# Router logits with the gate weights stationary, four token tiles at a time in quarters of the TensorE array

## What is computed

```python
# attention: 4 batches, 8 heads (4 local, 4 strided), 576 tokens each, head size 64
x = attention(q, k, v)                       # (2304 tokens, 512)
logits = x @ w_gate                          # w_gate is (512, 8)
logits = logits - logits.max()               # one maximum over all tokens and experts
P = np.exp(logits)
for _ in range(8):
    P /= P.sum(1, keepdims=True) + 1e-09
    P /= P.sum(0, keepdims=True) + 1e-09
    P *= N / E
for e in range(E):                           # 8 experts, 1024 wide
    out += P[:, e:e + 1] * (np.maximum(x @ w1[e], 0.0) @ w2[e])
return elu(out @ w_in) @ w_out               # 2048 wide
```

## Time and profile before

| What | us |
|---|---|
| median of 3 runs | 2053.81 (2052.08 to 2055.09) |
| the profiled execution | 2048.03 |
| span of its profile | 2046.2 |
| TensorE busy | 2020.0 (99% of the span) |
| VectorE, GpSimd, ScalarE busy | 1436.3, 1164.6, 903.0 |

### The profile page before, as it was taken

One profiled execution on the slowest core, in us unless ns is written; L12 is line 12 of the kernel. 1 busy time (PEld: TensorE's weight loads), 2 busy tenths in 40 slices (PEclk: granted clock), 3 DMA queues, 4 the chain that ended last, 5 costly groups with the idle time before them and its releaser, 6 DMA issues. The chain is left out here.

```text
span 2046.2 us, 29801 instructions
## 1 busy us (share of the span) xinstructions
PE 2020.0 (99%) x10611; PEld 1825.7 (89%) x10611; DVE 1436.3 (70%) x2462; ACT 903.0 (44%) x1659; POOL 1164.6 (57%) x1519
## 2 busy tenths in 40 slices
PE   7999999999999999999999999999999999999999
PEld 6889999999999999998999998999999999998988
DVE  5776877666667676666666778776666666778876
ACT  5763333333333343333333477433333333477775
POOL 3455755555555565555555567676555555657663
PEclk9999999999999999999999999999999999999999
DMA  7622212222221222212212221222122222221221
GB/s 138 132 63 73 73 62 62 73 72 62 66 79 62 62 64 81 63 62 73 73 62 63 72 72 63 93 72 73 62 62 78 67 62 73 73 63 62 93 73 52
DMA packets 159299, 147.69 MB, mean 72 GB/s; under 512 B 64432, under 2 KB 126128, under 8 KB 159152
## 3 DMA queue, kind: packets, MB, share of 16 engines
q1 hardware_dynamic: 159152, 145.79, 24.1%
HBM read 141.05 MB, written 4.72 MB: 71 GB/s over the span
## 5 line engine op out<-in xcount | busy, mean ns | idle before, releaser
L498 POOL TENSOR_TENSOR w_lo<-w_raw,w_hi 128x256 fp32r<-128x256 f32 x480 | 354.9, 770 | 750.5 <-ACT w_hi L847 750.5
L1116 DVE SCALAR_TENSOR_TENSOR acc<-psum,prob_eps,acc 128x512 f32<-128x512 f32 x516 | 387.0, 750 | 275.7 <-PE psum L722 269.1
L720 PE MATMUL psum<-w_hi,h_hi 128*128 128x512 f32 x1440 | 563.2, 391 | 0.6 <-issue 0.6
L722 PE MATMUL psum<-w_hi,h_lo 128*128 128x512 f32 x1440 | 563.3, 391 | 0.0
L721 PE MATMUL psum<-w_lo,h_hi 128*128 128x512 f32 x1440 | 561.3, 390 | 0.0
L661 PE MATMUL psum<-x_hi_a,w_hi 128*128 128x384 f32 x1296 | 438.4, 338 | 4.2 <-DVE c L1083 3.5
L664 PE MATMUL psum<-x_hi_a,w_lo 128*128 128x384 f32 x1296 | 438.3, 338 | 0.0
L663 PE MATMUL psum<-x_lo_a,w_hi 128*128 128x384 f32 x1296 | 437.0, 337 | 0.0
L491 POOL TENSOR_TENSOR w_lo<-s_tmp,w_hi 128x256 fp32r<-128x256 f32 x480 | 357.7, 776 | 0.0
L722 PEld LDWEIGHTS psum<-w_hi,h_lo 128*128 128x128 f32 x1440 | 270.3, 188 | 58.1
L720 PEld LDWEIGHTS psum<-w_hi,h_hi 128*128 128x128 f32 x1440 | 270.3, 188 | 43.9 <-issue 0.9
(11 more groups left out here) (118 smaller groups left out, 2743.0 us busy)
## 6 DMA issues: line engine op xcount, KB each, us to landing
w_raw<-in_moe_w_dram SPq DMA_DIRECT2D x192, 512.0 KB, 3.6
w_raw<-in_moe_w_in_dram SPq DMA_DIRECT2D x24, 512.0 KB, 3.4
w_raw<-in_moe_w_out_dram SPq DMA_DIRECT2D x24, 512.0 KB, 3.7
v_l<-in_v_dram SPq DMA_DIRECT2D x24, 128.0 KB, 3.6
out_dram<-acc SPq DMA_DIRECT2D x2, 1536.0 KB, 6.2
raw_l_q<-in_q_dram SPq DMA_DIRECT2D x8, 288.0 KB, 5.1
raw_l_k<-in_k_dram SPq DMA_DIRECT2D x8, 288.0 KB, 5.8
raw_s_q<-in_q_dram SPq DMA_DIRECT2D x16, 144.0 KB
```

The source lines that it names most:

```text
L498: pool.tensor_tensor(w2_lo[n % 2][piece], w2_raw[piece], w2_hi[n % 2][piece].bitcast(f32), ALU.subtract).then_inc(w2_lo_s, 1)
L720: pe.matmul(dst, h_hi[:, i, kk, js], w2_hi[s][:, i, :], start=(i == 0), stop=False)
L722: mm = pe.matmul(dst, h_lo[:, i, kk, js], w2_hi[s][:, i, :], start=False, stop=(i == 1))
L1116: ins = dve.scalar_tensor_tensor(a, y, 1.0 if bare else gate_of(n, j), a, ALU.mult, ALU.add)
```

## The change

`gate_raw` becomes `gate_pad`: each chunk's 8 gate columns with 24 zero columns beside them, so 32. `logit_round(r)` takes four token tiles at a time (the last round two). For each feature chunk it issues one matmul per tile, all with the same 128x32 block of `gate_pad` as the stationary operand and the tile's 128x128 of `xT` streamed past it; tile j writes partitions 32j to 32j+31 of one 128-column stretch of the `AUX` bank, which sets it to quarter j of the array's columns. The result is the transposed logits. ScalarE copies it to `logits_t` (`logit_copy`), and `select_logits(r)` turns it back with one matmul, `logits_t` stationary and chosen columns of the identity streamed, into the same columns of `AUX` as before. 18 tiles become 5 rounds: at steps (1, 4), (2, 4), (3, 4), with their selections at (1, 5), (2, 5), (3, 5), and two late ones. Three more edits: the gate's load waits for a memset of `gate_pad`, `make_t(0, 2)` waits for two rounds rather than six tiles, and `top_to_row` stands behind `p7(0)`.

```diff
+    QUARTER = P // 4
+    ROUNDS = -(-TT // 4)
...
-        gate_raw = sb("gate_raw", [P, DC, E], f32)
+        gate_pad = sb("gate_pad", [P, DC, QUARTER], f32)
+        logits_t = sb("logits_t", [P, 2, P], f32)
...
+        LOGIT_AT = {(1, 4): 0, (2, 4): 1, (3, 4): 2}
+        SELECT_AT = {(1, 5): 0, (2, 5): 1, (3, 5): 2}
+        LOGIT_LATE = range(len(LOGIT_AT), ROUNDS)
...
-                    sp.dma_start(gate_raw[:, :, :], w_gate.rearrange("(c p) e -> p c e", p=P)).then_inc(gate_in, 16)
+                    sp.wait_ge(gate_zeros, 1)
+                    sp.dma_start(gate_pad[:, :, 0:E], w_gate.rearrange("(c p) e -> p c e", p=P)).then_inc(gate_in, 16)
...
-                        pool.wait_ge(logit_ps, GT)
+                        pool.wait_ge(logit_t, -(-GT // 4))
...
-            def logit(tt, batch):
-                pe.wait_ge(x_done, GROUPS * (batch + 1))
+            def logit_round(r):
+                pe.wait_ge(x_done, GROUPS * -(-(4 * r + round_tiles(r)) * P // S))
+                dst, _ = logit_views(r)
                 for c in range(DC):
-                    mm = pe.matmul(bank(AUX)[:, tt * E:(tt + 1) * E], xT[:, c, tt * P:(tt + 1) * P],
-                                   gate_raw[:, c, :], start=(c == 0), stop=(c == DC - 1))
-                mm.then_inc(logit_ps, 1)
+                    for j in range(round_tiles(r)):
+                        t0 = (4 * r + j) * P
+                        mm = pe.matmul(dst[j * QUARTER:(j + 1) * QUARTER, :], gate_pad[:, c, :], xT[:, c, t0:t0 + P],
+                                       start=(c == 0), stop=(c == DC - 1))
+                mm.then_inc(logit_t, 1)
+
+            def select_logits(r):
+
+                pe.wait_ge(logit_copied, ROUNDS if r in LOGIT_LATE else r + 1)
+                n = round_tiles(r)
+                chosen = ident[0:QUARTER * n, 0:QUARTER * n].rearrange("p (j e) -> p j e", j=n)[:, :, 0:E]
+                pe.matmul(bank(AUX)[:, 4 * r * E:(4 * r + n) * E].rearrange("p (j e) -> p j e", e=E), logit_views(r)[1],
+                          chosen, start=True, stop=True).then_inc(logit_ps, 1)
...
-            for tt in LOGIT_LATE:
-                logit(tt, B - 1)
+            for r in LOGIT_LATE:
+                logit_round(r)
             p2(0)
+            for r in LOGIT_LATE:
+                select_logits(r)
+            p7(0)
             top_to_row()
-            p7(0)
             p4(0)
...
+            def logit_copy(r):
+                act.wait_ge(logit_t, r + 1)
+                if r not in LOGIT_LATE[1:]:
+                    wait(act, logit_ps, r)
+                src, dst = logit_views(r)
+                act.activation(dst, src, ACT.Copy).then_inc(logit_copied, 1)
...
                 if n < U:
                     snap(n)
+                if u == -1:
+                    for r in LOGIT_LATE:
+                        act.wait_ge(logit_t, ROUNDS)
+                        logit_copy(r)
```

More of the change, by code:

```diff
@@ L220, in build @@
         x_done = sem("x_done")
+        gate_zeros = sem("gate_zeros")
+        logit_t = sem("logit_t")
+        logit_copied = sem("logit_copied")
         logit_ps = sem("logit_ps")
@@ L290, in build, with round_tiles, logit_views @@
         W0_S, W0_HI_A, W0_HI_S, W0_LO_A, W0_LO_S = (3, 3), (3, 3), (3, 4), (3, 4), (3, 5)
-        LOGIT_AT = {}
-        tt = 0
-        for b in range(B - 1):
-            g = 5
-            while (tt + 1) * P <= (b + 1) * S:
-                LOGIT_AT[b + 1, g] = tt
-                tt, g = tt + 1, g + 1
-        LOGIT_LATE = range(tt, TT)
+        LOGIT_AT = {(1, 4): 0, (2, 4): 1, (3, 4): 2}
+        SELECT_AT = {(1, 5): 0, (2, 5): 1, (3, 5): 2}
+        LOGIT_LATE = range(len(LOGIT_AT), ROUNDS)
+        def round_tiles(r):
+            return min(4, TT - 4 * r)
+        def logit_views(r):
+            rows = QUARTER * round_tiles(r)
+            late = r - LOGIT_LATE[0] if r in LOGIT_LATE else 0
+            return bank(AUX)[0:rows, (2 + late) * P:(3 + late) * P], logits_t[0:rows, late, :]
         def x_splits(n):
@@ L434, in _ @@
             pool.memset(ones[:, :], 1.0).then_inc(ones_made, 1)
+            pool.memset(gate_pad[:, :, :], 0.0).then_inc(gate_zeros, 1)
             pool.memset(prob_eps[:, 0:TT, E:E + 1], EPS).then_inc(eps_made, 1)
@@ L747, in _ @@
                     fill(*f)
-                if (b, g) == (1, 5):
+                if (b, g) == (1, 4):
                     pe.wait_ge(gate_in, 16)
+                if (b, g) in SELECT_AT:
+                    select_logits(SELECT_AT[b, g])
                 if (b, g) in LOGIT_AT:
-                    logit(LOGIT_AT[b, g], b - 1)
+                    logit_round(LOGIT_AT[b, g])
                 if (b, g) == (B - 1, GROUPS):
@@ L913, in _ @@
                     exps(b, g)
+                if (b, g) in LOGIT_AT:
+                    logit_copy(LOGIT_AT[b, g])
                 if (b, g) in X0_HI:
@@ L1183, in _ @@
                 if u == -1:
-                    dve.wait_ge(logit_ps, TT)
+                    dve.wait_ge(logit_ps, ROUNDS)
                     dve.tensor_copy(logits[:, :, :], bank(AUX)[:, 0:TT * E].rearrange("p (t e) -> p t e", e=E))\
```

## The result

| What | before | after |
|---|---|---|
| median of 12 runs each, us | 2050.28 (2047.89 to 2055.09) | 2054.68 (2052.04 to 2060.70) |
| the profiled execution | 2048.03 | 2053.71 |
| span of its profile | 2046.2 | 2051.9 |
| from the first to the last copy or sum of a down projection | 1870.66 | 1876.24 |

The ratio, with its 95% interval in brackets, is 1.0024 [1.0015, 1.0032]: the changed kernel is slower by a quarter of a per cent, where I had forecast 0.22% faster.

A forecast was written before the change was run, and what follows sets the result against it. TensorE was taken as the bound from 180 us, so an earlier start would reach the end in full. Gains of 2.4 us (attention) and 2.2 us (behind it) sum to 4.6: 2053.81 to 2049.2 us, range 2045.8 to 2052.5.

The forecast's parts named there:

- the slower one: Router rounds: quarters run one after another and the clock falls in them; 2056.7 us, or 2065 at worst; chance 0.05.
- The attention's 2.4 us: Attention: three tiles removed from (3, 6) to (3, 8) gain 2.5 us, less 0.1 us for the selection's wait.
- The growing wait at (1, 9): Attention, batch 1: TensorE reaches strided v earlier, so its 0.44 us wait becomes 1 to 2 us; gain 0.
- The selection at (3, 5): Attention, batch 3: waits for ScalarE's copy behind the exponential of (3, 4), ends at about 131.1; cost 0.1 us.
- R: Length of the late rounds behind the attention, 48 records; taken as 3.0 us, bounds 1.75 and 5.2.
- Rival 1: Router rounds: four quarters run at once, R = 1.75; gain 5.8 us, 2048.0 us; chance 0.2.
- Rival 2: Router rounds: quarters run one after another, R = 5.2; gain 2.0 us, 2051.8 us; chance 0.2.
- `p4(0)` at R + 5.5: Behind the attention: p4(0) starts 5.5 us plus R after the late rounds start, held by VectorE's queue; before, 10.86 us.
- The idle 0.7 us: Behind the attention: TensorE stands idle 0.7 us before top_to_row, until VectorE's copy and maximum end at R + 3.4.
- The 0.2 us for changes of shape: Behind the attention: three changes between array shapes, 0.1 us each or less, cost 0.2 us in all.
- The cover of `p6(1)`: Behind the attention: GpSimd's splits end at R + 8.2, p6(1) comes at R + 9.2, leaving 1 us.
- Rival 3: Behind the attention: the clock falls anyway, costing 1.5 us; gain 3.1 us, 2050.7 us; chance 0.12.

The follow-up runs named there:

- the new tiles last: Changed kernel with gate_pad and logits_t declared behind all other tiles and 128 unused bytes in gate_raw's place; 2043.45 us, ratio 0.9970.
- the serial run: Kernel with the new tiles last, matmuls of feature chunks 1 to 3 all sent to the first quarter of the array; 2047.53 us, ratio 0.9988.
- The run with the reordered queue: Against the best one: VectorE's logits copy and maximum ahead of split_w1_a(1), make_u3(0) ahead of the row's maximum; 2041.49 us, ratio 0.9954.
- the padded one: Changed kernel with 640 unused bytes behind its new tiles, so later tiles move by 2048 bytes in all; 2044.25 us, ratio 0.9966.
- the best one: Kernel with the new tiles last, plus 160 unused bytes ahead of the attention's tiles alone; 2039.66 us, ratio 0.9946.
- the round one: Raw q and k and local v at multiples of 2048 bytes; first run: the new tiles last, all later tiles 160 bytes further, 2045.87 us, ratio 0.9981.

## Why the prediction was wrong, and where it was right

**The step that failed** stands in its first paragraph: "Nothing of the change lies there. Whatever start that stretch gets, earlier or later, reaches the end of the kernel in full". The second sentence held. The first did not: the operands of that stretch lie there, and the change moved them. I priced instructions and waits, counted the new tiles' memory nowhere, and took the pace of 4128 matmuls in 820 us as given. It was 4119: 5.6 us of the 5.69. None of the five rivals had it, not even the slower one, so the range missed the true side altogether. That the rest of the sum came near the router's own gain does not save it.

**The same omission in the attention**: "It waits on nothing that the router makes". That is so for these loads, and yet SyncE's chain became 3.5 us longer (133.79 against 130.26) by where it writes: the same shift of the attention's tiles in the kernel before gives 134.00. The attention's 2.4 us did not come: late 153.85 and 155.07 in the changed kernel, against 152.55 and 153.81 before. With the addresses put back they start at 151.05 and 150.76, so 1.5 to 3.1 us earlier; the forecast lies inside. The growing wait at (1, 9), 1.03 us, and the new one at (2, 9), 1.52, were forecast, but in the changed kernel late loads feed them too; with the new tiles last they are 1.22 us each. The masks of (3, 7) to (3, 9), where the gain was to come from, start behind 0.17, 0 and 0.23 us of idle time instead of 0.96, 0.80 and 0.90. The selection at (3, 5), at 133.33, stands behind 1.19 us of idle time. Its row names VectorE, but the code lets it wait for ScalarE's copy alone, and that ends at 133.27, right behind the exponential of (3, 4), as I had reckoned:

```profile
133.02 0.25 ACT L856 ACTIVATE logits_t<-psum 128x128 f32<-128x128 f32 x1
```

**R, the late rounds: mis-sized.** Forecast 3.0 us, measured 1.87; a full round 2.0 against 1.01. Rival 1, four quarters at once (1.75 and 0.87), was the right mechanism. I had taken the pace of four transposes, 0.0625 us a record, as the fastest possible; the rounds ran at 0.032 to 0.039. Rival 2, one after another, is refuted by these 1.87 us; the serial run shows its price, 0.111 us a record (I had 0.109). The Trainium skill (TensorE: Matmul & The Clock Gate, Part 3, Measured speedup vs the span model) gives 2.38 for three column tiles. The trace has 2.8 for a mix of four and two, so the page pointed the right way where my nearest row did not.

**Behind the attention: right but for two signs.** VectorE's queue is the end, and its order is as written. After, with late at 153.85:

```profile
158.08 0.30 DVE L1227 COPY logits<-psum 128x144 f32<-128x144 f32 x1
...
159.08 0.28 DVE L1232 TENSOR_REDUCE top_all<-psum 1x1 f32<-1x128 f32 x1 [0.36 <-PE psum L667]
...
159.88 0.55 DVE L1111 TENSOR_TENSOR c<-psum,c 128x384 f32<-128x384 f32 x1
```

`p4(0)` at R + 5.5 was forecast; it came at R + 4.85, mostly since the copy of the logits ended at R + 2.66 rather than R + 3.1. With R smaller as well, 10.86 became 6.72: 4.1 us won, forecast 2.2. The idle 1.6 us was 1.53. The idle 0.7 us ahead of `top_to_row` did not come: it starts at 158.77, 0.36 us behind the last matmul of `p7(0)`. The 0.2 us for changes of shape had no row with such a change behind it. The first matmul behind the late rounds is followed after 0.28 us where 0.175 is usual, and so is the first one behind the selections, which fill all columns, so no price of the change itself shows. The cover of `p6(1)`, "down to 1 us, but holds", held with less: in the second trace of the changed kernel GpSimd ends at 164.93 and `p6(1)` starts at 165.53. The run with the reordered queue took the rest of it.

**Rival 3, the clock, was underrated.** That PEclk stays at 1.00 from 150 to 165 us was one of the signs, and it did not. The clock fell behind the attention in one of two traces of the changed kernel, in that with the new tiles last (for 3.4 us) and the padded one (6.8 us), and not in the best one. So it is a matter of the execution as much as of the kernel. I had priced it at 1.5 us; the two traces of the changed kernel put it at 3.0. In both traces of the kernel before it lasts 6.8 us too.

**Sum.** The router's own part, with its neighbours left where they were, is 0.30% or 0.34% faster, some 6 to 7 us against the forecast 4.6. What lies above 4.6 comes from R, put 1.1 us too high, and `p4(0)` 0.65 us sooner behind the rounds than written. The shift costs 0.4 to 0.6%, more than the router gives, and the net is the 0.24% measured. The base was off as well: the forecast of 2049.2 us starts from 2053.81, the median of three, and twelve gave 2050.28, so the forecast gain alone would have led to 2045.7, just under the range. That error has nothing to do with the mechanism; the sign went wrong by the one term that was not in the sum.

**Open.** Which pair of tiles must lie how is not known: I moved groups of tiles, not single ones. What inside the chip makes the offset matter, for the matmuls or for the loads, was not tried. For the loads the offset's period was not measured either; the old placement and one 2048 bytes further were good, the round one 2 to 3 us better, and the one 1408 bytes further bad. Why matmuls of 384 columns got a little faster where those of 512 got slower is open too.

## What to carry to other kernels

An edit that adds or resizes a tile moves every tile declared behind it. Before judging it, run a control with the old code and the same number of unused bytes, and put new tiles last or pad them so that the others keep their offset (here multiples of 256 bytes left the pace of the matmuls alone, and 2048 bytes in all restored both losses). Where TensorE is busy all the time, compare the count of matmuls in a fixed stretch, as the busy share cannot fall. And a thin cover named in a forecast, like the 1 us of `p6(1)`, is the first thing to look at before moving another piece of work beside it.

## What the runs showed of the hardware

- Where the expert stage's tiles lie changes the pace of its matmuls. The mean step from one start to the next, from 180 us on, is 228.2 ns for 512 columns and 176.4 to 176.7 for 384 at the old place, also with 256, 512 or 1024 bytes added; in the four traces with 1408 bytes added it is 230.3 and 175.7 to 175.9.
- SyncE's time to issue one load of local v has a median of 506 to 508 ns in twelve traces with the attention's tiles at their old place, 2048 bytes further or on round addresses, and 543 in a thirteenth (the serial quarters). In the four traces with these tiles shifted by 1408 bytes it is 590 to 642 ns. The 20 strided loads took 15.4 to 16.3 us in either kind.
- Float32 matmuls in four quarters of the array's columns overlap: 1.01 us for 32 records of 128 streamed columns that cost 0.111 us each one after another, 3.5 times as fast; with half of the sets only two wide, 2.8 times.
- The granted clock fell to 1.2 GHz, or did not, behind the same 1.5 us of idle time in different executions of the same program.
